# A linear-attention, mixture-of-experts and feed-forward kernel: each attention load waits for its own buffer, the first expert's weights come in six pieces, and a logit sum is computed two units earlier

## The reference

```python
# attention: B, H, S, D = 4, 8, 768, 48
for t in range(S):
    state = alpha[:, :, t, :, None] * state + np.einsum('bhd,bhe->bhde', k[:, :, t], v[:, :, t])
    y[:, :, t] = np.einsum('bhd,bhde->bhe', q[:, :, t], state)
x = y.transpose(0, 2, 1, 3).reshape(B * S, H * D)          # 3072 x 384
# expert layer: 8 experts, each token goes to one
logits = xn @ en.T / tau                                   # xn, en: rows divided by their norm
expert_idx = argmax(logits);  gate_w = softmax(logits)[expert_idx]
out[mask] = gate_w[mask, None] * (np.maximum(x[mask] @ w1[e], 0.0) @ w2[e])   # w1 384x1024, w2 1024x384
# feed-forward
h = np.maximum(np.maximum(x @ w1, x @ w2), x @ w3);  out = h @ w_out          # 384x768, 768x384
```

## Time and profile before

| | |
|---|---|
| time, median of 3 runs | 779.61 us (778.14 to 781.35) |
| the profiled execution's time | 779.84 us |
| its span, first to last instruction | 778.1 us |
| PE busy over the span | 718.1 us (92%) |
| DVE, ACT, POOL busy | 366.9, 260.5, 294.5 us |
| PE busy in the first 200 us | 154.17 us |
| PE busy from 200 us to the end | 563.89 us of 578.10 |
| mean granted TensorE clock | 0.974 |

### The profile page before, as it was taken

How to read it: one execution, slowest core, us unless ns; L and a number is a source line. 1 busy time by engine, 2 the same in 40 slices (tenths; PEclk the granted TensorE clock), 3 DMA queues, 4 the chain that set the end, 5 groups by cost and what they waited for, 6 DMA issues and landing times.

```text
span 778.1 us, 16539 instructions
## 1 busy us (share of the span) xinstructions
PE 718.1 (92%) x5510; PEld 634.2 (82%) x5511; DVE 366.9 (47%) x688; ACT 260.5 (33%) x635; POOL 294.5 (38%) x232
## 2 busy tenths in 40 slices
PE   5299999972899999999999999999999999999995
PEld 5298888861699999999998887888888888888885
DVE  7389898857733343342433148323333333233321
ACT  4378898843222222222222221211111111112110
POOL 4044454301464484545457678023033131320011
PEclk9699999995999999999999999999999999999999
DMA  9967878206490624515242020001001010000001
GB/s 191 270 128 159 182 167 159 78 3 225 165 344 24 211 112 134 211 53 191 71 163 80 34 74 21 21 30 42 11 32 51 10 41 30 20 20 1 11 21 51
DMA packets 128804, 74.71 MB, mean 96 GB/s; under 512 B 103448, under 2 KB 122016, under 8 KB 128736
## 3 DMA queue, kind: packets, MB, share of 16 engines
q1 hardware_dynamic: 116896, 53.22, 25.4%
q10 hardware_dynamic: 7744, 10.38, 3.7%
q0 software_dynamic: 4096, 10.24, 3.5%
HBM read 59.03 MB, written 14.79 MB: 95 GB/s over the span
## 4 chain that ended last, share of the span: by engine, by line
PE 76%; issue 11%; DMA 4%; SPq 3%; DVE 3%; POOL 1%; ACT 1%; POOLq 0%; DVEq 0%; ACTq 0%
PE bank L1455 56%; PE bank L1259 3%; DMA nat<-in_alpha 3%; PE bank L1491 3%; SPq L305 3%; PE bank L1345 3%; PE bank L1297 3%; PE bank L1354 2%; PE bank L1307 2%; PE bank L1333 1%; PE bank L1441 1%; POOL out L550 1%; PE bank L1286 1%; PE bank L1513 1%; DVE low1h L1074 1%
## 5 line engine op out<-in xcount | busy, mean ns | idle before, releaser
L510 POOL TENSOR_TENSOR wsp<-raw,wsp 128x1536 f32 x28 | 103.4, 3714 | 92.2 <-DVE wsp L1139 92.1
L1455 PE MATMUL bank<-yh,mh 128*128 128x512 f32 x324 | 128.2, 396 | 0.1
L1455 PE MATMUL bank<-yh,ml 128*128 128x512 f32 x324 | 126.5, 390 | 0.0
L550 POOL DMA_INDIRECT out<-oo,tok_t x24 | 24.2, 1009 | 202.9 <-DVE oo L1196 202.9
L1455 PE MATMUL bank<-yl,mh 128*128 128x512 f32 x324 | 91.4, 390 | 0.0
L1455 PE MATMUL bank<-wsp,xh 128*128 (+1 forms) x324 | 85.3, 398 | 3.9 <-issue 3.3
L1455 PE MATMUL bank<-wsp,hTh 128*128 x432 | 81.8, 340 | 0.0
L841 ACT CAST gh<-t 128x512 fp32r<-128x512 f32 x36 | 22.3, 620 | 155.5 <-DVE t L1207 155.5
L1455 PEld LDWEIGHTS bank<-wsp,hTh 128*128 128x128 f32 x432 | 73.9, 188 | 0.2 <-issue 0.2
L1455 PEld LDWEIGHTS bank<-wsp,xh 128*128 128x128 f32 x324 | 58.9, 188 | 16.0 <-issue 4.3
L1455 PEld LDWEIGHTS bank<-yl,mh 128*128 128x128 f32 x324 | 60.8, 188 | 13.0
(11 more groups left out here) (209 smaller groups left out, 1251.5 us busy)
## 6 DMA issues: line engine op xcount, KB each, us to landing
raw<-in_moe_w SPq DMA_DIRECT2D x16, 1536.0 KB, 8.2
expert_rows<-ye ACTq DMA_DIRECT2D x27, 193.0 KB
yg<-expert_rows SPq DMA_DIRECT2D x24, 193.0 KB
nat<-in_k SPq DMA_DIRECT2D x32, 144.0 KB, 3.2
nat<-in_q SPq DMA_DIRECT2D x32, 144.0 KB, 3.0
vt<-in_v SPq DMA_DIRECT2D x32, 144.0 KB, 2.8
attention_rows<-xc SPq DMA_DIRECT2D x4, 1152.0 KB, 5.1
nat<-in_alpha SPq DMA_DIRECT2D x30, 144.0 KB, 2.9
```

The costliest lines, as they stand in the source:

```text
L510: g.tensor_tensor(wsp[:, ds(to, 1), 1, n, part], raw[:, n:n + 1, part], wsp[:, ds(to, 1), 0, n, part].bitcast(f32), ALU.subtract).then_inc ...
L550: g.indirect_dma_start(out=out, out_offset=bass.IndirectOffsetOnAxis(ap=tok_t[:, i, 0:1], axis=0), in_=oo[i % 2][:], in_offset=None).then_ ...
L1455: last = mm(o, x, y, start=(n == 0), stop=(n == len(todo) - 1))
```

## The change

The change has three parts. SP's queue is written anew: each of alpha, k, q and v follows the event that frees its own buffer (`pe_a`, `pe_k`, `pe_q`, `pe_Y`), and the stores stand one or two iterations later. The first expert's weights are loaded in six pieces, one after every second iteration, and GpSimd's splits move from u = 0 to 11 to u = 2 to 13, in a loop that is unrolled. The logit sum goes into VectorE's `step(13)`, and the two instructions of the count into `step(14)`.

```diff
-    w0_in, w0_hi, w0_lo = new("w0_in", "w0_hi", "w0_lo")
+    w0_in = new(*[f"w0_in{i}" for i in range(6)])
+    w0_hi, w0_lo = new("w0_hi", "w0_lo")
@@ SP @@
         def store_x(b):
 
             sp.wait_ge(act_X, CR + 8 * b + 8)
+            if b:
+                sp.wait_ge(x_out, CR + 16 * b)
...
-        for j, n in ((0, 0), (0, 1), (0, 2), (2, 0), (1, 1), (1, 2), (0, 3),
-                     (3, 0), (2, 1), (1, 3), (2, 2), (2, 3), (3, 1), (3, 2), (3, 3)):
+        w0_parts = [(0, c, 1) for c in range(KD)] + [(1, 0, 3), (1, 3, 3), (1, 6, 2)]
+
+        def load_w0(i):
+
+            n, k0, count = w0_parts[i]
+            m = (F, DM)[n]
+            sp.dma_start(raw0[:, n, m * k0:m * (k0 + count)].rearrange("p (k m) -> p k m", m=m),
+                         kd((w1, w2)[n][0])[:, k0:k0 + count, :]).then_inc(w0_in[i], 16)
+
+        for j, n in ((0, 0), (0, 1), (0, 2), (2, 0), (1, 1), (0, 3), (3, 0)):
             load_one(j, j, n)
-        for n in range(2):
-            sp.dma_start(raw0[:, n, :].rearrange("p (k m) -> p k m", m=(F, DM)[n]), kd((w1, w2)[n][0])
-                         ).then_inc(w0_in, 16)
-        for u in range(NU - UPB):
-            j = u % UPB
-
-            sp.wait_ge(pe_q, 2 * u + 2)
-            for n in range(3):
-                load_one(u + UPB, j, n)
-            sp.wait_ge(pe_Y, CR + 2 * u + 2)
-            load_one(u + UPB, j, 3)
-            if u and j == 0:
-                store_x(u // UPB - 1)
+        for m in range(NU - 1):
+            if m + 4 < NU:
+                sp.wait_ge(pe_a, 2 * m + 2)
+                load_one(m + 4, m % UPB, 0)
+            if m >= 3:
+                sp.wait_ge(pe_q, 2 * (m - 3) + 2)
+            load_one(m + 1, (m + 1) % UPB, 2)
+            if m + 2 < NU:
+                if m >= 2:
+                    sp.wait_ge(pe_k, 2 * (m - 2) + 2)
+                load_one(m + 2, (m + 2) % UPB, 1)
+            if m >= 3:
+                sp.wait_ge(pe_Y, CR + 2 * (m - 3) + 2)
+            load_one(m + 1, (m + 1) % UPB, 3)
+            if m % 2 == 0 and 2 <= m < 2 + 2 * len(w0_in):
+                load_w0(m // 2 - 1)
+            if m % UPB == 0 and m >= 2 * UPB:
+                store_x(m // UPB - 2)
@@ GpSimd @@
-        with pool.Fori(0, B - 1) as b:
-            for j in range(UPB):
-                decay(UPB * b + j + 2, (j + 2) % UPB)
-                pool.wait_ge(w0_in, 32)
-
-                pool.wait_ge(dve_w, CR + UPB * b + j + 3)
-                part = ds(W0 * (UPB * b + j), W0)
-                split(hi0_f[:, part], lo0_f[:, part], raw0_f[:, part], w0_hi, w0_lo, UPB * b + j + 1)
-        for u in range(NU - UPB, NU - 2):
+        for u in range(NU - 2):
             decay(u + 2, (u + 2) % UPB)
+            if u >= 2:
+                if u % 2 == 0:
+                    pool.wait_ge(w0_in[u // 2 - 1], 16)
+
+                pool.wait_ge(dve_w, CR + u + 3)
+                part = slice(W0 * (u - 2), W0 * (u - 1))
+                split(hi0_f[:, part], lo0_f[:, part], raw0_f[:, part], w0_hi, w0_lo, u - 1)
@@ VectorE, step(u) @@
             states(u, j)
+            if u == NU - 3:
+                sum_logits(0, B - 1)
+            if u == NU - 2:
+
+                dve.wait_ge(act_r, NU)
+                dve.wait_ge(act_sumA, CR + NU)
+                link(d.tensor_scalar(fits[:], sums[:], LIMIT, None, ALU.is_lt))
+                d.tensor_reduce(good[:], fits[:].rearrange("p a u -> p (a u)"), AX.X, ALU.add).then_inc(fl_good, 1)
             if u + 3 < NU:
                 scans(u + 3, (j + 3) % UPB)
...
-        for j in range(UPB):
-            if j == UPB - 1:
-                sum_logits(0, B - 1)
-
-                dve.wait_ge(act_r, NU)
-                dve.wait_ge(act_sumA, CR + NU)
-                link(d.tensor_scalar(fits[:], sums[:], LIMIT, None, ALU.is_lt))
-                d.tensor_reduce(good[:], fits[:].rearrange("p a u -> p (a u)"), AX.X, ALU.add).then_inc(fl_good, 1)
-            step(NU - UPB + j)
+        for u in range(NU - UPB, NU):
+            step(u)
```

More of the change, by code:

```diff
@@ L942, in states, with sum_logits @@
                                        bank[4][:, D * c:D * c + D], ALU.mult, ALU.add).then_inc(dve_st, 1)
+        def sum_logits(b0, b1):
+            dve.wait_ge(act_X, CR + 8 * b1)
+            link(d.tensor_reduce(lg[:, CH * b0:CH * b1, :],
+                                 lgp[:, CH * b0:CH * b1].rearrange("p t j e -> p t e j"), AX.X, ALU.add))
         def step(u):
```

## The result

| | |
|---|---|
| changed kernel, median of 4 runs | 760.9 us (759.91 to 764.01) |
| kernel before on the same chip, median of 4 runs | 780.48 us (778.14 to 783.14) |
| ratio | 0.9755, 95% interval 0.9712 to 0.9798 |
| profiled execution, span | 760.82 us, 759.1 us |
| PE busy over the span | 716.8 us (94%) |

What follows compares the result with a forecast made beforehand. TensorE's own work was taken to set the pace in attention, leaving only its idle time and slow clock to win back. 12.8 + 2.6 + 4.4 = 19.8 us less gave 759.8 us, range 756.5 to 766.0.

Steps and rivals of the forecast that it cites:

- The long wait: Behind unit 0, TensorE's 12.22 us wait for unit 4's alpha goes; unit 1's scores start at 28.5, gaining 12.8 us.
- Two short waits: TensorE's waits for alpha at 83.11 and 118.87 us, behind stores, both go: 2.6 us gained (0 to 2.6).
- Units of 8.64 us throughout, with PEclk 1.00: Profile sign: every attention unit takes 8.64 us, with TensorE's clock at its upper level from 24 to 160 us.
- The logit sum: At attention's end, moving sum and count lets unit 15 start earlier at the upper clock: 4.4 us gained (3.3 to 4.9).
- The 0.1 allowed: Allowance in us because the 2.21 us logit sum fits VectorE's 2.23 us idle gap with 0.02 to spare.
- DMA engines keep up: Over four attention units, 27.9 to 33.8 us of DMA work fits in 34.6 us, so cost nothing.
- DMA paces some units: Rival, 13%: load groups among pieces and stores cost 1.75 us, not 1.40, giving 765, at worst 770 us.
- the one of a slower kernel: Rival, 3%: in the middle units SP's queue makes DMA set the pace and all gains are lost, about 784 us.
- Pieces and splits at nothing: Six weight pieces and GpSimd's splits in units 2 to 13 were taken to cost nothing in the attention stage.
- The estimate of 3.8 us: Time of one weight piece at 138 GB/s; four units would then take 36 us, 1.4 more than TensorE needs.
- About 20 earlier and otherwise the same: Profile sign: from the first expert tile on, everything shifts about 20 us earlier and is otherwise unchanged.

Runs made afterwards that it cites:

- b_store_later: Kernel before with only the stores of batches 0 and 1 moved behind the loads of one unit later: 779.79 us, ratio 1.0009.
- the second profile: Profile of the changed kernel run once more, unaltered, as base for other experiments: 761.72 us, ratio 0.9747 to the kernel before.
- b_logits_only: Kernel before with only the logit sum moved to step 13 and the count to step 14: 772.54 us, ratio 0.9924.
- a_two_weights: Changed kernel with the weights in two whole loads, in iterations 2 and 6, in place of six pieces: 758.69 us, ratio 0.9719.
- a_pool_early: Changed kernel with GpSimd's splits left in units 0 to 11, each waiting for its piece: 765.35 us, ratio 0.9789.

## Why the prediction was right, and where it was not

- **The long wait: 12.8 forecast, 13.17 measured.** The queue works as described, alpha 4 is there in time, the clock stays up. ScalarE's three checks were indeed what is late next. Only the waiter was misread: it is not the copy of alpha 4 for `turn_kp(1)` (26.70 + 0.87) but the copy of y, for which the transposes of unit 2's k wait (1.25 us at 26.57). Both are behind the same three checks, so the number came out. And 0.38 of the 13.17 us come from ahead of the wait: unit 0's last products start at 22.57 in place of 22.95.
- **Two short waits: 2.6 forecast, 2.61 measured, and 3.70 lost beside it.** This is the step that failed: "Both short waits go" was right, but the store's cost did not go with them. Moved by about a unit, the store meets TensorE's instruction packet in place of alpha. b_store_later is the clean case: both waits gone, ratio 1.0009. "Units of 8.64 us throughout, with PEclk 1.00" was wrong in unit 10 and, in the second profile, in unit 6 as well.
- **The logit sum: 4.4 forecast, 4.88 measured** (3.56 + 1.32), at the upper bound of 4.9; b_logits_only shows it alone. `lg` took 2.29 us in a gap of 2.23, and cost unit 14 nothing: its scores start 7.97 us after unit 13's in both traces (147.08 and 155.05, 135.00 and 142.97). The 0.1 allowed was not needed.
- **DMA engines keep up: right.** Their share is 0.98 to 1.12 for long stretches, and no load is waited for. The rival "DMA paces some units" and the one of a slower kernel found nothing in the traces.
- **Pieces and splits at nothing: half right.** Pieces against whole loads are nothing (a_two_weights, 0.9719 both). The Trainium skill's rule on small transfers (DMA: Bandwidth & Descriptors, section Bandwidth), by which the pieces were the wrong direction, shows in no time here: the lead hides what it may cost. (The estimate of 3.8 us took the page's rate for 64 KB for pieces of 512 KB, and so was a high one.) That the splits cost nothing in units 2 to 13 was right. But their place is worth 3.6 us (a_pool_early), which the term passed over: it only looked at the load of GpSimd, and did not ask what the splits would do at u = 0 and 1 with the pieces not yet there.
- **"About 20 earlier and otherwise the same" from the first expert tile on:** the expert stage starts 16.78 us earlier (199.96 to 183.18). 13.17 + 2.61 + 4.88 = 20.66 would have been 0.9 above the forecast's 19.8; the gap took 3.70, and the missing collision of VectorE and GpSimd gave some 2 back in this execution. That the total (19.0 by the spans, 19.6 by the medians) came so near 19.8 is thus in part luck.

How the parts stand together: alone on the kernel before, weights, store and logit sum give by their ratios 1.9 - 0.7 + 5.9 = 7.1 us, and the change 19.1 (0.0245 of 780.5). I put the other 12 us down to the lead itself, with each buffer filled as soon as it is free; no run had the new queue alone, with the weights where they were, so this is what is left over, not a measurement.

## What to carry to other kernels

When a wait behind a large load is to go, give the queue a lead first: moving the load moves the wait to the next victim. A transfer moved off one wait can land on the instruction stream of the busiest engine; look for idle time marked "issue" in the middle of a group of matmuls, and shift the transfer by a unit or a few us. And judge a helper engine's new place not by its load but by what it waits for and which instructions of its neighbour it then falls on.

## What was not expected of the hardware

- Packets of instructions of about 0.02 MB come by DMA while the kernel runs, most of them 4 to 9 us apart; in the eleven cases in which one came 9.9 to 11.7 us after the last, TensorE stood idle for 0.65 to 2.22 us.
- Behind gaps of 1.75, 2.00 and 2.22 us the 18 transposes were slow (3.85, 3.83 and 2.91 us in place of 2.18), but not behind one of 2.03 (a_pool_early, 2.19), nor behind any of 1.46 or less.
- Beside GpSimd's splits six VectorE scans took 5.47 us in place of 2.0 to 2.4, and one `gl` 2.25 in place of 0.69.
- The DMA engines' share stood at 1.03 with 203 GB/s over a whole unit without a wait of TensorE: a full share says nothing on whether anybody is late.
